# Eight experts written out without a loop, gate products moved among the last dense blocks, and an alternating order of the two layers' products

## The reference, cut to what matters

```python
x = attention(q, k, v, beta)                   # 3072 tokens x 384, untouched by the change
h = x @ w_in                                   # dense stage, 384 -> 2048
g = h * tanh(softplus(h))
x = g @ w_out                                  # 2048 -> 384
P = exp(x @ w_gate - max)                      # 3072 x 8, the gate
for _ in range(8):                             # eight Sinkhorn rounds
    P /= P.sum(1, keepdims=True) + 1e-9
    P /= P.sum(0, keepdims=True) + 1e-9
    P *= N / E
for e in range(8):                             # eight experts, all tokens
    out += P[:, e:e+1] * (relu(x @ w1[e]) @ w2[e])
```

## Time and profile before

| | |
|---|---|
| median of three runs | 2540.57 us |
| the profiled execution | 2541.44 us |
| its span | 2539.3 us |
| PE busy | 2458.4 us, 97% |
| DVE, ACT, POOL busy | 1295.7, 871.6, 436.0 us |
| mean granted TensorE clock | 0.972 |
| dense stage, first product | 533.9 us from the span's start |
| first gate product | 937.5 us |
| first expert product | 945.8 us |

### The profile page before, as it was taken

How to read it: one execution, slowest core, us unless ns; L and a number is a source line. 1 busy time by engine, 2 the same in 40 slices (tenths; PEclk the granted TensorE clock), 3 DMA queues, 4 the chain that set the end, 5 groups by cost and what they waited for, 6 DMA issues and landing times.

```text
span 2539.3 us, 39851 instructions
## 1 busy us (share of the span) xinstructions
PE 2458.4 (97%) x15288; PEld 2070.6 (82%) x15288; DVE 1295.7 (51%) x2426; ACT 871.6 (34%) x1894; POOL 436.0 (17%) x356
## 2 busy tenths in 40 slices
PE   6989889989999999999999999999999999999999
PEld 5889888878888868888887887887887887888887
DVE  5766557668777764443333333333333333333344
ACT  5867567846666641111111111111111111111111
POOL 7665556400000021100000000000000000000000
PEclk8988779989999999999999999999999999999999
DMA  1110010020000010101101101001011011011013
GB/s 62 43 44 23 23 44 23 17 75 26 0 0 0 0 31 27 44 9 50 42 10 46 42 13 47 28 27 43 9 50 43 9 46 43 13 46 42 17 25 71
DMA packets 58885, 79.34 MB, mean 31 GB/s; under 512 B 37584, under 2 KB 38352, under 8 KB 56656
## 3 DMA queue, kind: packets, MB, share of 16 engines
q1 hardware_dynamic: 54256, 63.33, 8.0%
q10 hardware_dynamic: 4464, 13.50, 1.5%
HBM read 71.81 MB, written 5.01 MB: 30 GB/s over the span
## 4 chain that ended last, share of the span: by engine, by line
PE 74%; issue 2%; DVE 2%; ACT 0%; POOL 0%; DMA 0%; DVEq 0%; ACTq 0%; POOLq 0%
PE ex_h L52 37%; PE ex_y L52 37%; DVE de_hg L770 0%; DVE de_en L757 0%; DVE de_g_lo L750 0%; DMA de_stage<-w_in 0%; POOL ex_w_lo L1002 0%; DVE de_en L755 0%; ACT de_g_hi L703 0%; DVE de_w_lo L739 0%; DVE ex_term L1115 0%; POOL ex_col L1021 0%; DVE ex_acc L1129 0%; PE ex_logits L52 0%; DVE ex_row L1079 0%
## 5 line engine op out<-in xcount | busy, mean ns | idle before, releaser
L1161 DVE SCALAR_TENSOR_TENSOR ex_r_lo<-ex_h,ex_r_hi 128x512 fp32r<-128x512 f32 x384 | 264.1, 689 | 939.3 <-ACT ex_r_hi L1049 939.2
L1049 ACT ACTIVATE ex_r_hi<-ex_h 128x512 fp32r<-128x512 f32 x384 | 229.9, 599 | 1309.7 <-PE ex_h L52 1309.7
L52 PE MATMUL ex_h<-x_lo,ex_w_hi 128*128 128x512 f32 x1152 | 449.9, 391 | 11.9 <-issue 11.9
L52 PE MATMUL ex_y<-ex_r_hi,ex_w_hi 128*128 128x512 f32 x1152 | 449.6, 390 | 1.7 <-DVE ex_r_lo L1161 1.7
L52 PE MATMUL ex_h<-x_hi,ex_w_lo 128*128 128x512 f32 x1152 | 450.0, 391 | 0.0
L52 PE MATMUL ex_h<-x_hi,ex_w_hi 128*128 128x512 f32 x1152 | 449.7, 390 | 0.1
L52 PE MATMUL ex_y<-ex_r_lo,ex_w_hi 128*128 128x512 f32 x1152 | 449.4, 390 | 0.0
L52 PE MATMUL ex_y<-ex_r_hi,ex_w_lo 128*128 128x512 f32 x1152 | 449.4, 390 | 0.0
L1002 POOL TENSOR_TENSOR ex_w_lo<-ex_stage,ex_w_hi 128x512 fp32r<-128x512 f32 x96 | 124.0, 1292 | 1340.7 <-ACT ex_w_hi L1033 1305.3
L52 PEld LDWEIGHTS ex_h<-x_hi,ex_w_lo 128*128 128x128 f32 x1152 | 217.0, 188 | 58.0 <-issue 12.9
L52 PEld LDWEIGHTS ex_y<-ex_r_hi,ex_w_hi 128*128 128x128 f32 x1152 | 217.1, 188 | 47.4 <-DVE ex_r_lo L1161 2.1
(11 more groups left out here) (136 smaller groups left out, 3346.4 us busy)
## 6 DMA issues: line engine op xcount, KB each, us to landing
ex_stage<-w_exp SPq DMA_DIRECT2D x16, 1536.0 KB, 6.4
ex_pb<-p_rows SPq DMA_DIRECT2D x90, 256.0 KB, 3.4
at_qT<-q_t ACTq DMA_DIRECT2D x10, 512.0 KB, 4.1
at_v_in<-v ACTq DMA_DIRECT2D x11, 384.0 KB, 3.1
at_k_in<-k ACTq DMA_DIRECT2D x10, 384.0 KB, 4.7
out<-ex_stage SPq DMA_DIRECT2D x60, 64.0 KB, 1.9
de_stage<-w_in SPq DMA_DIRECT2D x8, 384.0 KB, 3.3
de_stage<-w_out SPq DMA_DIRECT2D x8, 384.0 KB, 3.2
```

Source lines behind the costliest of these rows:

```text
L52: return nc.tensor.matmul(out, lhsT, rhs, start=start, stop=stop)
L1049: nc.scalar.activation(r[0][:, j, :], h_bank[j][:], ACT.Relu).then_inc(hi_ready, 1)
L1161: nc.vector.scalar_tensor_tensor(out=r[1][:, j, :], in0=h_bank[j][:], scalar=0.0, in1=r[0][:, j, :].bitcast(F32), op0=ALU.max, op1=ALU.sub ...
```

## The change

The loop over experts becomes plain Python, so all eight are written out for each engine, and the second multiplication of `ex_acc` at the end of expert 0 is dropped (the steps now know which expert came before).

The gate products of token block 0 to 3 go in front of the last three second-layer blocks of the dense stage; those of block 4 and 5 follow it. The copy to `ex_w_hi` of the first half moves from POOL to ACT, in the hook of chunks 6, 7, 8, 10, 11 and 12 of the last dense token block; the load of its weights is cut in two DMAs.

SH becomes 1. DVE's slots move from before L1161 of j = 0 and 2 to behind L1161 of j = 3 and 1, which with the new SH is the same place in DVE's order for the same slot. POOL's two slots of step n are now 2n-1 and 2n, ahead of split(n).

In the steps' chunks j = 0, 1 and 3, three products of the first layer and three of the second alternate. At j = 2 the order stays.

```diff
-            expert(0)
-            with eng.Fori(1, E - 1) as e:
+            for e in range(E):
                 expert(e)
-            expert(E - 1)
...
-    SH = 2
+    SH = 1
+    FIRST = (6, 7, 8, 10, 11, 12)
...
             real, count = past(tb, f, LAG)
+            if not new:
+                tail(f)
...
+            sp.wait_ge(*dense.h_read(DF // 4))
+            sp.dma_start(stage[:, 0:GW], w_exp[0, 0][:, 0:GW]).then_inc(w1_staged, 16)
             sp.wait_ge(*dense.h_read(DF // 2))
-            sp.dma_start(stage[:], w_exp[0, 0]).then_inc(staged0, 16)
+            sp.dma_start(stage[:, GW:2 * GW], w_exp[0, 0][:, GW:2 * GW]).then_inc(w2_staged, 16)
...
-            pool.wait_ge(staged0, 16)
-            pool.wait_ge(*dense.w2_read(DF // 2))
             for i in range(PIECES):
-                cols = slice(i * PW, (i + 1) * PW)
-                nc.gpsimd.tensor_copy(w[0][0][:, cols], stage[:, cols]).then_inc(whi_ready, 1)
+                if i % (PIECES // 2) == 0:
+                    pool.wait_ge(*dense.w2_read(DF // 2 if i else DF // 4))
                 split(0, 0, i)
...
+                if f in FIRST:
+                    split(0, 0, FIRST.index(f))
...
                 for j in range(FC):
-                    if first(e) and j % 2 == 0:
-                        sinkhorn(2 * (g * NB + tb) + j // 2 - SH)
                     dve.wait_ge(hi_ready, n * FC + j + 1)
...
+                    if first(e) and j % 2 == 1:
+                        sinkhorn(2 * (g * NB + tb) + j // 2 - SH)
...
+            def gating(tb):
+                if tb == 0:
+                    pe.wait_ge(glo_ready, 1)
+                elif tb <= FC:
+                    pe.wait_ge(*dense.h_taken(tb))
+                pe.wait_ge(*dense.x_split(tb))
...
+            def before_dense_tail(f):
+                gating(f)
+                if f == 2:
+                    gating(3)
+
+            dense.pe(pe, before_dense_tail)
+            gating(NB - 2)
+            gating(NB - 1)
...
-                    last.then_inc(h_done, 1)
-                    if j >= LAG:
-                        down(e, g, tb, j - LAG)
-                    elif not (first(e) and g == 0 and tb == 0):
-                        down(*previous(e, g, tb), j - LAG + FC)
+                        if m == MC - 1:
+                            last.then_inc(h_done, 1)
+                        if j > LAG:
+                            down(e, g, tb, j - LAG, [m])
+                        elif j < LAG and not (first(e) and g == 0 and tb == 0):
+                            down(*previous(e, g, tb), j - LAG + FC, [m])
+                    if j == LAG:
+                        down(e, g, tb, 0)
```

More of the change, by code:

```diff
@@ L782, in dve_program, with pe_program @@
         run(dve, step)
-    def pe_program(pe):
+    def pe_program(pe, tail):
         def step(tb, f, new):
@@ L822, in dense_programs @@
     return Dense(sp_program, pool_program, act_program, dve_program, pe_program,
-                 h_read, w2_read, (hn_ready, NB * FC), lambda tb: (xlo_ready, (tb + 1) * MC))
+                 h_read, w2_read, lambda n: (hn_ready, NB * FC - R + n), lambda tb: (xlo_ready, (tb + 1) * MC))
 def dense_and_experts_phase(nc, w_in, w_out, w_gate, masks, w_exp, out, x_hi, x_lo, MC, N, F1, E, F):
@@ L887, in dense_and_experts_phase @@
         gate_loaded, ident_loaded, ghi_ready, glo_ready = s.sems("gate_loaded ident_loaded ghi_ready glo_ready")
-        staged0, staged, whi_ready, wlo_ready = s.sems("staged0 staged whi_ready wlo_ready")
+        w1_staged, w2_staged, staged, whi_ready, wlo_ready = s.sems("w1_staged w2_staged staged whi_ready wlo_ready")
         gated, gated_ready = s.sems("gated gated_ready")
-        h_done, hi_ready, lo_ready, y_done, term_ready, rescaled, acc_ready = s.sems(
-            "h_done hi_ready lo_ready y_done term_ready rescaled acc_ready")
+        h_done, hi_ready, lo_ready, y_done, term_ready, acc_ready = s.sems(
+            "h_done hi_ready lo_ready y_done term_ready acc_ready")
         lg_stored, lg_loaded, logits_ready, top_ready, alltop_ready, negtop_ready, prob_ready = s.sems(
@@ L906, in dense_and_experts_phase, with run @@
         turn = stage[:].rearrange("p (b m t) -> p b m t", b=2, m=MC)
-        def run(eng, step, tail=None):
+        def run(step, tail=None):
             def expert(e):
@@ L956, in load_pb @@
                     sp.wait_ge(acc_ready, (n - RB + 1) * MC)
-                sp.dma_start(pb[:, tb % RB, :], p_rows[bass.ds(e, 1), tb * TB:(tb + 1) * TB].to_broadcast([P, TB])).then_inc(
+                sp.dma_start(pb[:, tb % RB, :], p_rows[e:e + 1, tb * TB:(tb + 1) * TB].to_broadcast([P, TB])).then_inc(
                     pb_loaded[tb % RB], 16)
@@ L992, in tail @@
                 sp.wait_ge(last_stored, 16 * TC)
-            run(sp, step, tail)
+            run(step, tail)
         @block.gpsimd
@@ L1023, in step @@
                     split(e + g, 1 - g, tb)
-            run(pool, step)
+            run(step)
         @block.scalar
@@ L1029, in split @@
             def split(e, g, i):
-                if i == 0:
+                if first(e) and g == 0:
+                    if i % (PIECES // 2) == 0:
+                        act.wait_ge(w2_staged if i else w1_staged, 16)
+                elif i == 0:
                     act.wait_ge(staged, 16 * (2 * e + g))
@@ L1043, in step @@
                 n = steps_before(e, g, tb)
-                if first(e) and g == 0 and tb == 1 + SH // 2:
+                if first(e) and g == 0 and tb == 2:
                     act.wait_ge(negtop_ready, 1)
@@ L1059, in tail @@
                     nc.scalar.copy(out_last[:, t], h_bank[t][:, 0:DM]).then_inc(act_out, 1)
-            run(act, step, tail)
+            run(step, tail)
         @block.vector
@@ L1187, in tail @@
                     nc.vector.tensor_copy(out_last[:, t], h_bank[t][:, 0:DM]).then_inc(dve_out, 1)
-            run(dve, step, tail)
+            run(step, tail)
         @block.tensor
         def _(pe):
[L1194 to L1197, removed]
+            def gating(tb):
[3 more added lines that the diff above has]
+                    pe.wait_ge(*dense.h_taken(tb))
                 pe.wait_ge(*dense.x_split(tb))
@@ L1251, in tail @@
                             last.then_inc(last_turned, 1)
-            run(pe, step, tail)
+            run(step, tail)
 def build(nc, q_t, k, v, beta, masks, w_in, w_out, w_gate, fold, w_exp, out, B, H, S, D, F1, E, F2):
```

## The result

The changed kernel takes 2526.99 us (median of 4 runs, 2523.36 to 2530.43), the kernel before 2540.88 beside it (4 runs, 2539.12 to 2541.25). The ratio is 0.9947, with the 95% interval 0.9929 to 0.9964: 13.9 us faster, 15.9 were forecast. The profiled execution of the changed kernel took 2530.43 us, span 2528.6, mean granted clock 0.974.

A forecast was written before the change was run, and what follows sets the result against it. PE was taken as the bound. 18.2 + 3.9 + 2.0 - 8.0 - 0.2 = 15.9 us off the profiled 2541.44 gave 2525.5; that execution lay 0.87 above the median, so 2524.7 was predicted, range 2515 to 2532.

The forecast's parts named there:

- The loop: Five hardware-loop returns between experts: PE's stops and lower clock there vanish when code is written out; gain 18.2 us.
- the late piece: Expert 0: split(5) on POOL comes later, so PE stands 6.3 us, plus 1.7 for lower clock; loss 8.0 us.
- The rival of stops at the experts' beginnings: Stops remain where each expert begins, as code fetched late; 2542.9 us, no change; chance 0.07.
- The end of the dense stage: Last dense blocks and gate products: PE's lost time shrinks though POOL still delays the ACT and DVE chain; gain 3.9 us.
- The old stop: Expert 0: PE's wait of 1.7 us for the hidden tile's low part goes; gain 2.0 us.
- The alternating order: Experts' steps: bank slack shrinks from 1.9 to 0.5 us and holds; only the last chunk is late; loss 0.2 us.

The follow-up runs named there:

- The loop alone: Kernel before, with the loop over experts written out and the second multiplication of `ex_acc` dropped, nothing else: 2522.49 us, ratio 0.9937.
- The best version: Changed kernel, with expert 0's first-half low weight pieces made on DVE and POOL's L1004 in the dense stage waiting for L770: 2512.79 us, ratio 0.99.
- the gate products alone: Kernel before, with only the gate products moved among the last dense blocks; POOL still makes both kinds of pieces: 2541.02 us, ratio 1.0005.
- POOL's slots as before: Changed kernel, with POOL's slots 2n-2 and 2n-1 ahead of split(n) again and DVE's order left: 2522.04 us, ratio 0.9926.

## Why the prediction was right, and where it was off

**The loop, 18.2: shown.** The trace of after has no "issue" stop, and products keep their 0.2263 us. The loop alone gave 15.85 us with a stop for `ex_r_lo` that cost 2.34 more, together 18.2. The best version agrees: its expert stretch lacks the loop, the stop of 2.0 and the late piece, and 1593.46 - 18.2 - 2.0 + 0.2 = 1573.46 by my terms stands against 1573.64. The rival of stops at the experts' beginnings is out.

**The end of the dense stage, 3.9: the size holds (3.68, in the dense end 3.73), its reason only in part.** The chain went as I wrote: L770 at 1.67 in most of the six chunks, 0.99 us more, the Exp of chunk 15 at 930.07 where 927.3 plus the trace's shift of 2.66 makes 929.96. But the gate products alone, with twelve operations of POOL, gave 3.3 of the 3.7. So moving the casts to ACT earned 0.4 us between these traces: six operations spread over six chunks, each just ahead of L770, delay the chain nearly as much as twelve did. Part of the gate products' own gain I had not seen, and it looks like luck: before, a stop for `de_g_lo` that ends at 920.94 is followed by a stretch at the lower clock; in the kernel with the gate products alone, the stretch behind the like stop (it ends at 919.89) kept the full one. The stop and the stretch of the kernel before, and then of the one with the gate products alone:

```profile
920.94 0.47 PE L52 MATMUL ex_y<-de_g_hi,de_w_hi 128*128 128x512 f32 x1 [1.92 <-DVE de_g_lo L750]
...
922.05:925.04 2.99, 2.99 (x8) 0.50 0.00 0
```

```profile
919.89 0.47 PE L52 MATMUL ex_y<-de_g_hi,de_w_hi 128*128 128x512 f32 x1 [1.91 <-DVE de_g_lo L750]
...
919.90:923.00 3.10, 3.10 (x14) 1.00 0.00 0
```

Eight products in 2.99 us, where the full clock makes thirteen, is some 1.2 us. With the loop alone, the clock fell behind this stop too. So in two traces of three it fell there, and the one in which it did not is the one with the gate products alone. Without that luck the gate products would have earned some 2.1 us (2.4 expected) and the casts 1.6: how the 3.7 divide between the two is not settled. The changed dense stage has no stop of that length, and its traces show no such stretch.

The Trainium skill's rule on the shared port ("SBUF — State Buffer", section "Who interferes with whom": whole instructions exclude each other and issue order decides) is borne out. L770 has both inputs in SBUF and lost 0.99; when POOL was held until it had passed, it kept 0.68 and the dense end fell by 2.6 (2.7 expected).

**The old stop, 2.0: gone**, by POOL's slot order: with the old order the waits for `ex_r_lo` are back (4.7 us in three, which with the clock behind the last cost 1580.88 - 1573.68 = 7.2), and with the loop alone one stayed (2.4, cost 4.3).

**The late piece, 8.0: the mechanism as forecast, the size too small; this is the step that was off.** It measured 10.1 (8.15 standing, 1.97 at half clock). Round 2's all-reduce came at S + 48.54 (forecast 48.5). The turns took 55.0 us instead of 3 x 17.76 = 53.3, so split(5) ended at S + 112.2 instead of S + 110.4. I had read the length of a turn from one pair of rows. A change of kind is not of one length: in this stretch of after it is 6.96 to 7.38 us towards the weight piece and 5.82 to 6.28 back. Other traces of the same order waited 7.3, 6.8 and 5.7. That the slot order makes this stop is shown from two sides: it goes when the order is put back, and it goes when POOL has no pieces to make.

**The alternating order, 0.2: the trace says 0.4.** Besides the end, it puts round 2's row part 1.36 later, which I had counted into the late piece. Blocks stayed at 2.04 us, so the change of bank every three products costs PE nothing that can be seen. The bank held, with 0.46 us to spare where I had 0.5.

**Sum.** By measured terms, 18.2 + 3.7 + 2.0 - 10.1 - 0.4 = 13.4 us. The two stretches of the traces lost 3.68 + 9.68 = 13.36, and the medians are 13.9 apart. The forecast was 15.9; nearly all of the difference is the late piece.

## What to carry to other kernels

Before an engine's program is reordered, count the engine's changes between kinds of work, not only its operations: here one place in POOL's order moved a stop of 10 us onto PE. Where the slower engine shares a port with the engine on the critical chain, one wait that lets the chain's operation pass first (here 2.6 us) can be worth more than moving work away (0.4 to 1.6 us). And test the parts of a bundle alone: the loop by itself was at least as fast as the whole change, the alternating order gave nothing, and POOL's new slot order took more than it gave (2.9 us of the expert stretch by its own experiment).

## What the runs showed of the hardware

**At a hardware loop's return PE stood 2.1 to 2.6 us each time** with a body of 195.8 us, and up to 3.1 in a program that differs only outside the loop; with the lower clock behind some of them the five cost 18.2 us, 3.6 each. Code written out for eight experts ran without a stop.

**POOL pays for a change between all-reduce and elementwise work** with 5.5 to 7.7 us, and in each of the four traces with the old slot order one change takes 8.7 to 9.3 (9.27 in the kernel before, 8.97 with the loop alone, 8.74 with POOL's slots as before, and 8.85 with the gate products alone, shown here). Each time it is the change behind split(5), just after SP has issued the next load of 1.5 MB. That the load is the cause was not tried and stays open.

```profile
1043.70 1.28 POOL L1004 TENSOR_TENSOR ex_w_lo<-ex_stage,ex_w_hi 128x512 fp32r<-128x512 f32 x1 [6.81 <-issue]
1053.84 0.43 POOL L1023 PARTITION_ALL_REDUCE ex_col<-ex_col  x1 [8.85 <-issue]
```

**The same stop may or may not be followed by the lower clock.** Two stops of 1.92 and 1.91 us, in the same place of two kernels, were followed by a granted clock of 0.50 and of 1.00 (rows above). The stops for `ex_r_lo` in expert 0 were followed by the lower clock at 2.4 us (the loop alone), and not at 1.7 (before). The one of 8.0 us was followed by 4.01 us at 0.50.
